# The second batch's gate products, moved from two blocks at the end of attention into slots of its last four steps

## The chip, the cores and the metric

The kernel runs on one core of one Trainium2 chip. The metric is the device time in microseconds of one execution. Before the change it is 691.11 us, the median of three runs (688.9 to 693.77).

## The reference, cut to what matters

Three layers follow one another: banded attention with four sink positions, a mixture of experts whose tokens are assigned greedily by gate logit, and a gated product.

```python
scores = scale * q @ k.T                       # B=2, H=8, S=768, D=64, window 128, 4 sinks
a = softmax(where(keep, scores, -1e9))
x = (a @ v)  -> (B*S, H*D) = (1536, 512)
logits = x @ w_gate                            # 512 x 8
# all (token, expert) pairs in order of falling logit; an expert takes 1536/8 = 192 tokens
out[mask_e] = relu(x[mask_e] @ w1[e]) @ w2[e]  # F = 1024
return ((y @ w_a) * (y @ w_b)) @ w_out         # d_ff = 1536
```

The logits need all 512 columns of a token's x, that is all four head pairs of its batch, and the assignment needs the logits of every token.

## The kernel before, in words

Attention is a loop over 48 steps, `t` from 0 to 47: 2 batches x 4 head pairs x 6 blocks of 128 queries. Head pair `g = t // 6` runs from 0 to 7; the last one, 7, is batch 1, pair 3, steps 42 to 47. Every engine has its own hand-ordered copy of this loop. On TensorE (`@block.tensor`) one turn `t` holds `transposes(t)` (the softmax rows of step t, L1222 and L1225), `scores(t + 2)` (L1209, absent in turns 46 and 47), `side_jobs(t, 0)`, `values(t - 1)` (eight records from L1244 and two from L1249: a 32-bit float product is two records of matmul and two of weight load), and `side_jobs(t, 1)`. A last turn 48 holds only `values(47)` and side jobs. VectorE finds the maxima of the scores (L761), copies half of the transposes (L791) and scales the values into `x_rows` (`keep_x`, L800). ScalarE takes the exponentials (L595), and copies the other half (L606, L610).

Side jobs are work for the next pair or for the gate. `side_list()` gives each a turn `t`, a place (0 ahead of `values`, 1 behind it), a kind and a half of the batch's 768 tokens. The kinds:

- `k`, `q`: turn the next pair's keys and queries (L1186).
- `rows`: turn three 128x128 tiles of `x_rows` with TensorE into bank 7 (L1276); ScalarE copies them to `xT` (L623).
- `gate`, `logits`: the first batch's product, `wg` (512x8) as the stationary operand and 384 columns of `xT` moving, then three small transposes back. They are not touched.
- `direct`: the second batch's product (L1258), `xT` tiles of 128x128 as the stationary operand and eight columns of `wg` moving. A half has three token tiles and four blocks of 128 input columns (one per head pair), 12 products in all; half 0 sums in bank 0, half 1 in bank 1. VectorE copies each half to `L` (L818).

The two semaphores `side_ready` (TensorE to the reader) and `side_done` (reader to TensorE) count the jobs in the order of the list; TensorE waits for `side_done` of every earlier job before it starts one, since they share bank 7. `SIDES` is their number.

At the end of attention before the change: `direct` half 0 stands in turn 47 behind `values(46)` with all 12 products, and right behind it TensorE issues the first three blocks of half 1, 9 products, without a wait. That is one run of 21 products ahead of `values(47)`. Turn 48: `values(47)`, `rows` of pair 7 half 1, then `direct` half 1 with the last block, three products.

Behind this the routing begins. VectorE waits for `side_done` = `SIDES`, sums `|L|` (L899), and runs a chain with small products on TensorE (L1324, L1332, L1336), which ends in the token order; GpSimd gathers the rows by it, and TensorE starts the experts (L1406, L1407). GpSimd's constants (L502 to L509) and two weight loads on SyncE (L400, expert 1, units 2 and 3) also wait for `SIDES`. SyncE stores `x_rows` of each pair (L394).

Of the kernel before, what the change touches and what calls it, by code (L numbers as in the profile page):

```python
# [5 lines left out]
def attention_moe_gated_product_kernel(  # L6
# [17 lines left out]
    ACT = mybir.ActivationFunctionType  # L24
    AX = mybir.AxisListType

    P = 128
# [3 lines left out]
    E = w_gate.shape[1]  # L31
# [5 lines left out]
    NBLK = S // P  # L37
    NPAIR = H // 2
    NCH = N // P
    KD = DM // P  # L40
# [31 lines left out]
    with ctx:  # L72
# [3 lines left out]
        def sem(name):  # L76
            return ctx.enter_context(nc.semaphore(name))
# [14 lines left out]
        L = sb("L", [P, NCH, E], stack=early)  # L92
# [25 lines left out]
        xT = sb("xT", [P, KD, S], stack=attn)  # L118
        wg = sb("wg", [P, KD, E], stack=attn)
# [65 lines left out]
        bank = [psum[:, i, :] for i in range(8)]  # L185
# [18 lines left out]
        side_done = sem("side_done")  # L204
# [8 lines left out]
        pts_done = sem("pts_done")  # L213
        o_ready = sem("o_ready")
        x_kept = sem("x_kept")

        dve_step = sem("dve_step")
        abs_ready = sem("abs_ready")
# [53 lines left out]
        HS = S // 2  # L272
# [6 lines left out]
        STEPS_A = B * NPB  # L279
        PAIRS = B * NPAIR  # L280

        def side_list():

            jobs = []
            for g in range(PAIRS):
                t = NBLK * g
                if g + 1 < PAIRS:
                    jobs += [(t + 1, 1, "k", g + 1, 0), (t + 2, 0, "k", g + 1, 1),
                             (t + 2, 1, "q", g + 1, 0), (t + 3, 0, "q", g + 1, 1)]
                jobs += [(t + 4, 0, "rows", g, 0)]  # L290
                if g + 1 < PAIRS:
                    jobs += [(t + 7, 0, "rows", g, 1)]
                    if g % NPAIR == NPAIR - 1:
                        jobs += [(t + 6, 0, "gate", g, 0), (t + 9, 1, "logits", g, 0),
                                 (t + 11, 0, "gate", g, 1), (t + 12, 0, "logits", g, 1)]
            last = PAIRS - 1
            return sorted(jobs) + [(STEPS_A - 1, 1, "direct", last, 0), (STEPS_A, 1, "rows", last, 1),
                                   (STEPS_A, 1, "direct", last, 1)]

        SIDES = len(side_list())  # L300

        def side_number(kind, g, half):
            return [job[2:] for job in side_list()].index((kind, g, half))
# [152 lines left out]
        def _(pool):  # L456
# [41 lines left out]
                nc.gpsimd.tensor_tensor(ring_lo[u][:, :], raw[u][:, :], ring[u][:, :].bitcast(f32),  # L498
                                        ALU.subtract).then_inc(w_lo[u], 1)

            pool.wait_ge(side_done, SIDES)
            nc.gpsimd.memset(thr[:, 0, :], -BIG)  # L502
            nc.gpsimd.memset(thr[:, 1, :], 0.0)
            nc.gpsimd.iota(tid[:], pattern=[[P, NCH], [0, E]], base=1, channel_multiplier=1,
# [62 lines left out]
        def _(act):  # L567
# [45 lines left out]
            def side_jobs(t, late):  # L613
                for no, (at_t, at_late, kind, g, half) in enumerate(side_list()):
                    if (at_t, at_late) != (t, late) or kind not in ("k", "q", "rows"):
                        continue
                    act.wait_ge(side_ready, no + 1)
                    if kind == "k":
                        round_k(bank[7], g, half).then_inc(rounded, 1)
                    elif kind == "q":  # L620
                        round_q(bank[7], g, half).then_inc(rounded, 1)
                    else:
                        nc.scalar.activation(xT[:, g % NPAIR, half * HS:(half + 1) * HS], bank[7][:, 0:HS],  # L623
                                             ACT.Copy).then_inc(side_done, 1)

            def round_ahead(t):

# [103 lines left out]
        def _(dve):  # L731
# [72 lines left out]
            def side_jobs(t, late):  # L804
                for no, (at_t, at_late, kind, g, half) in enumerate(side_list()):
                    if (at_t, at_late) != (t, late) or kind == "rows":
                        continue
                    dve.wait_ge(side_ready, no + 1)
                    c0 = g // NPAIR * NBLK + 3 * half
                    if kind == "k":  # L810
                        split_k(bank[7], g, half, rounds_before(kind, g, half)).then_inc(side_done, 1)
                    elif kind == "q":
                        split_q(bank[7], g, half, rounds_before(kind, g, half)).then_inc(side_done, 1)
                    elif kind == "gate":
                        nc.vector.tensor_copy(LT[:, half * HS:(half + 1) * HS], bank[7][0:E, 0:HS]).then_inc(side_done, 1)
                    else:
                        src = bank[half] if kind == "direct" else bank[7]
                        nc.vector.tensor_copy(L[:, c0:c0 + 3, :], src[:, 0:3 * E].rearrange("p (i e) -> p i e", e=E)  # L818
                                              ).then_inc(side_done, 1)

            nc.vector.memset(spin[:], 1.0).then_inc(spin_ready, 1)
# [72 lines left out]

            dve.wait_ge(rconsts, 1)

            dve.wait_ge(side_done, SIDES)
            at(dve_step, 0)
            nc.vector.tensor_reduce(out=absum[:], in_=L[:], axis=AX.XY, op=ALU.add,  # L899
                                    apply_absolute_value=True).then_inc(abs_ready, 1)  # L900
# [3 lines left out]
            for d in range(1, E):  # L904
                op = nc.vector.tensor_tensor(ties[:, :, o:o + E - d], L[:, :, d:E], L[:, :, 0:E - d], ALU.is_equal)
# [17 lines left out]
            with dve.Fori(0, STEPS) as st:  # L923
# [12 lines left out]
                for c in range(NCH):  # L936

                    op = nc.vector.tensor_scalar(above[:, c, :], bucket[:], um[:, c:c + 1], None, op0=ALU.is_le)  # L938
# [51 lines left out]
            with dve.If(even_v == 0):  # L990
# [20 lines left out]
                with dve.Fori(0, ROUNDS) as r:  # L1011
# [9 lines left out]
                    for c in range(NCH):  # L1021
                        gb = c % 4
                        if c >= 4:
# [3 lines left out]
                        op = nc.vector.scalar_tensor_tensor(out=G[:, gb, own], in0=mrow[:, own],  # L1027
                                                            scalar=m[:, c:c + 1], in1=tielt[:], op0=ALU.subtract,
                                                            op1=ALU.is_lt)
                        if c > 0:  # L1030

                            op = nc.vector.tensor_scalar(G[:, gb, 0:c * P], mrow[:, 0:c * P], m[:, c:c + 1], None,
                                                         op0=ALU.is_lt)
                        if c < NCH - 1:
                            op = nc.vector.tensor_scalar(G[:, gb, (c + 1) * P:N], mrow[:, (c + 1) * P:N],
                                                         m[:, c:c + 1], None, op0=ALU.is_le)
# [140 lines left out]
        def _(pe):  # L1177
# [72 lines left out]
                                            skip_group_check=True)  # L1250
                last.then_inc(o_ready, 1)

            def direct(half, blocks):

                for t in blocks:
                    for i in range(3):
                        at = (3 * half + i) * P
                        op = nc.tensor.matmul(bank[half][:, i * E:(i + 1) * E], xT[:, t, at:at + P], wg[:, t, :],  # L1258
                                              start=(t == 0 and i == 0), stop=(t == KD - 1), skip_group_check=True)
                return op  # L1260

            def side_jobs(t, late):
                for no, (at_t, at_late, kind, g, half) in enumerate(side_list()):
                    if (at_t, at_late) != (t, late):
                        continue

                    if no == 0:
                        pe.wait_ge(first_lo, 4)
                    pe.wait_ge(side_done, no)
                    b, pr = divmod(g, NPAIR)  # L1270
                    hs = slice(half * HS, (half + 1) * HS)
                    if kind == "rows":

                        pe.wait_ge(x_kept, NBLK * g + 3 * half + 3)
                        for i in range(3):
                            op = nc.tensor.transpose(bank[7][:, i * P:(i + 1) * P],  # L1276
                                                     x_rows[:, b * NBLK + 3 * half + i, pr * P:(pr + 1) * P], ident[:])
                    elif kind == "gate":
                        if b == 0 and half == 0:
                            pe.wait_ge(wg_in, 16)  # L1280
                        for blk in range(KD):
                            op = nc.tensor.matmul(bank[7][0:E, 0:HS], wg[:, blk, :], xT[:, blk, hs], start=(blk == 0),  # L1282
                                                  stop=(blk == KD - 1))
                    elif kind == "logits":
                        for i in range(3):
                            op = nc.tensor.transpose(bank[7][:, i * E:(i + 1) * E],
                                                     LT[:, half * HS + i * P:half * HS + (i + 1) * P], ident[0:E, 0:E])
                    elif kind == "direct":
                        op = direct(half, range(KD) if half == 0 else range(KD - 1, KD))
                    else:  # L1290
                        if half == 0:
                            pe.wait_ge((q_in, k_in)[kind == "k"][pr], 32 * (b + 1))
                        op = transposed(bank[7], (q_raw, k_raw)[kind == "k"], pr, half)
                    op.then_inc(side_ready, 1)
                    if kind == "direct" and half == 0:
                        direct(1, range(KD - 1))

            pe.wait_ge(spin_ready, 1)
            spinning(14, bank[0])
# [13 lines left out]
            for t in range(1, STEPS_A + 1):  # L1313
# [5 lines left out]
                values(t - 1)  # L1319
                side_jobs(t, 1)  # L1320


            pe.wait_ge(abs_ready, 1)
            nc.tensor.matmul(bank[0][:, 0:1], ones[:], absum[:], start=True, stop=True).then_inc(abs_summed, 1)  # L1324
# [205 lines left out]
```

## Time and profile before

| what | us |
|---|---|
| median of three runs | 691.11 |
| the profiled execution, its own time | 689.06 |
| its span, first to last instruction | 687.3 |
| outside the span | 1.76 |
| attention, to the end of the last `values` | about 168 |
| routing, to the first expert product | about 168 to 231 |
| experts and gated product | 231 to 687 |

The span is what the profile shows in detail; the 1.76 us around it is taken as it is. "Granted clock" is the share of TensorE's full clock that it ran at in a stretch; its two levels here are 1.00 (2.4 GHz) and 0.50 (1.2 GHz). PE is the matmul row of TensorE and PEld its weight-load row. The end of a matmul is modelled, so the distance from one start to the next says more than the duration of one record.

### The profile page before, as it was taken

To read this page: it belongs to the slowest core of one execution; us is meant where nothing else is said; L and a number is where in the kernel's file an instruction comes from. 1 tells how busy PE (TensorE), PEld (TensorE's weight loads), DVE (VectorE), ACT (ScalarE), POOL (GpSimd) and SP (SyncE) were. 2 spreads that over 40 slices of the span, in tenths; PEclk is the share of its full clock that TensorE was granted. 3 is DMA by queue.
4 is the path that set the end of the run, shared out by engine and by line. 5 is a ranking of instruction groups with operands and counts; after the bars stand their busy time and mean duration, and the time that the engine had idled before them with its cause. 6 is when DMAs were issued, how large, how long until landed. Compare 5 with 4: busy or idle time off the path is not lost.

```text
span 687.3 us, 10549 instructions
## 1 busy us (share of the span) xinstructions
PE 622.6 (91%) x3666; PEld 529.3 (77%) x3666; DVE 328.6 (48%) x979; ACT 301.5 (44%) x685; POOL 136.8 (20%) x74
## 2 busy tenths in 40 slices
PE   7999999999212699999999999999999999999995
PEld 4877776788111699999999888888888888888884
DVE  4677656761886187777777522212221213222221
ACT  3676665660000177777777433323342415141411
POOL 3000000000000602222222005050613223441402
PEclk8999999996555699999999999999999999999999
DMA  9954150220300636766676505050604131523001
GB/s 191 265 130 92 48 169 24 85 87 23 122 0 3 184 95 214 233 207 233 244 229 199 184 0 184 0 184 2 242 17 166 51 132 61 183 73 110 0 0 61
DMA packets 85812, 81.22 MB, mean 118 GB/s; under 512 B 39697, under 2 KB 62225, under 8 KB 85777
## 3 DMA queue, kind: packets, MB, share of 16 engines
q1 hardware_dynamic: 83856, 74.49, 36.2%
q0 software_dynamic: 1920, 6.29, 2.7%
q8 instruction: 19, 0.31, 0.2%
q14 instruction: 17, 0.13, 0.1%
HBM read 74.48 MB, written 6.29 MB: 118 GB/s over the span
## 4 chain that ended last, share of the span: by engine, by line
PE 85%; DVE 8%; issue 2%; ACT 2%; POOL 1%; DMA 1%; DVEq 0%; ACTq 0%; POOLq 0%
PE psum L1406 15%; PE psum L1399 15%; PE psum L1400 14%; PE psum L1401 14%; PE psum L1407 7%; PE psum L1244 5%; PE psum L1222 3%; PE psum L1209 3%; PE psum L1249 2%; DVE above L938 2%; PE psum L1186 2%; PE psum L1258 1%; PE psum L1276 1%; PE psum L1390 1%; PE psum L1282 1%
## 5 line engine op out<-in xcount | busy, mean ns | idle before, releaser
L498 POOL TENSOR_TENSOR w_lo<-w_raw,w_hi 128x2048 fp32r<-128x2048 f32 x23 | 106.5, 4646 | 298.3 <-ACT w_hi L575 298.3
L575 ACT ACTIVATE w_hi<-w_raw 128x1024 fp32r<-128x1024 f32 (+1 forms) x126 | 123.5, 999 | 18.7 <-PE psum L1401 18.7
L1150 DVE TENSOR_TENSOR g_sb<-psum,a_sb 128x512 f32<-128x512 f32 x36 | 24.9, 692 | 197.0 <-PE psum L1401 197.0
L1399 PE MATMUL psum<-y_hi,w_hi 128*128 x288 | 113.1, 393 | 0.0
L1401 PE MATMUL psum<-y_hi,w_lo 128*128 x288 | 112.2, 389 | 0.0
L1400 PE MATMUL psum<-y_lo,w_hi 128*128 x288 | 112.1, 389 | 0.0
L735 DVE TENSOR_TENSOR w_lo<-w_raw,w_hi 128x1024 fp32r<-128x1024 f32 x64 | 77.8, 1215 | 0.0
L1406 PE MATMUL psum<-x_hl,w_hi 128*128 (+1 forms) x256 | 75.2, 365 | 1.6 <-DVE x_hl L1100 1.6
L1406 PE MATMUL psum<-h_hl,w_hi 128*128 128x384 f32 x256 | 74.6, 361 | 0.0
L1407 PE MATMUL psum<-x_hl,w_lo 128*128 (+1 forms) x256 | 64.7, 253 | 0.0
L1399 PEld LDWEIGHTS psum<-y_hi,w_hi 128*128 128x128 f32 x288 | 54.0, 188 | 13.5 <-POOL w_lo L498 2.5
L1407 PE MATMUL psum<-h_hl,w_lo 128*128 128x192 f32 x256 | 64.1, 250 | 0.0
L1401 PEld LDWEIGHTS psum<-y_hi,w_lo 128*128 128x128 f32 x288 | 54.1, 188 | 11.4
L708 ACT ACTIVATE g_hi<-g_sb 128x512 fp32r<-128x512 f32 x36 | 22.8, 632 | 91.1 <-DVE g_sb L1150 91.1
L1400 PEld LDWEIGHTS psum<-y_lo,w_hi 128*128 128x128 f32 x288 | 54.1, 188 | 11.0
L702 ACT ACTIVATE a_sb<-psum 128x512 f32<-128x512 f32 x36 | 21.5, 598 | 88.2 <-PE psum L1401 88.2
L1399 PE MATMUL psum<-w_hi,g_hi 128*128 128x512 f32 x144 | 56.9, 395 | 0.0
L1400 PE MATMUL psum<-w_lo,g_hi 128*128 128x512 f32 x144 | 56.1, 390 | 0.0
L1401 PE MATMUL psum<-w_hi,g_lo 128*128 128x512 f32 x144 | 56.0, 389 | 0.0
L595 ACT ACTIVATE p_sb<-psum,nmax 128x264 f32<-128x264 f32 (+1 forms) x96 | 43.4, 459 | 21.3 <-DVE nmax L761 21.3
L1406 PEld LDWEIGHTS psum<-x_hl,w_hi 128*128 128x128 f32 x256 | 48.9, 191 | 2.0 <-issue 2.0
L1407 PEld LDWEIGHTS psum<-x_hl,w_lo 128*128 128x128 f32 x256 | 49.7, 194 | 0.0
(154 smaller groups left out, 998.3 us busy)
## 6 DMA issues: line engine op xcount, KB each, us to landing
w_raw<-in_moe_w_dram SPq DMA_DIRECT2D x32, 1024.0 KB, 5.1
w_raw<-in_moe_w_a_dram SPq DMA_DIRECT2D x9, 1024.0 KB, 5.2
w_raw<-in_moe_w_b_dram SPq DMA_DIRECT2D x9, 1024.0 KB, 5.1
w_raw<-in_moe_w_out_dram SPq DMA_DIRECT2D x9, 1024.0 KB, 5.5
k_raw<-in_k_dram SPq DMA_DIRECT2D x16, 192.0 KB, 3.8
q_raw<-in_q_dram SPq DMA_DIRECT2D x16, 192.0 KB, 4.0
v_sb<-in_v_dram SPq DMA_DIRECT2D x16, 192.0 KB, 4.2
xs_scratch<-x_rows SPq DMA_DIRECT2D x8, 384.0 KB, 3.6
```

The source lines that it names most:

```text
L498: nc.gpsimd.tensor_tensor(ring_lo[u][:, :], raw[u][:, :], ring[u][:, :].bitcast(f32), ALU.subtract).then_inc(w_lo[u], 1)
L575: op = nc.scalar.activation(ring[slot][:, ps], raw[r][:, ps], ACT.Copy)
L595: op = nc.scalar.activation(p_sb[:, t % 2, h * SW:(h + 1) * SW][:, span(t, h)], bank[2 * (t % 2) + h][:, span(t, h)], ACT.Exp, scale=-1.0, ...
L708: nc.scalar.activation(g_hi[:, j % 2, :], g_sb[:, j % 2, :], ACT.Copy).then_inc(g_hi_done, 1)
L735: op = nc.vector.tensor_tensor(ring_lo[slot][:, hs], raw[slot][:, hs], ring[slot][:, hs].bitcast(f32), ALU.subtract)
L1150: nc.vector.tensor_tensor(g_sb[:, j % 2, :], bank[2 + j % 2][:, :], a_sb[:, j % 2, :], ALU.mult).then_inc(g_prod, 1)
L1244: last = nc.tensor.matmul(o[:, h * D:(h + 1) * D], pT[:, t % 2, blk, h, :], v_sb[:, pr, i - 1 + blk, h, :], start=(h == 0 and blk == t0), ...
L1399: nc.tensor.matmul(o, lhs_hi, rhs_hi, start=first, stop=False)
L1400: nc.tensor.matmul(o, lhs_hi, rhs_lo, start=False, stop=False)
L1401: return nc.tensor.matmul(o, lhs_lo, rhs_hi, start=False, stop=final)
L1406: nc.tensor.matmul(bk[:, 0:2 * CAP], lhs_hi, rhs_both, start=first, stop=False)
L1407: return nc.tensor.matmul(bk[:, 0:CAP], lhs_lo, rhs_hi, start=False, stop=final)
```

## The change

The 24 products stay, with the same operands. What changes is where they stand and where they sum:

- All 24 sum in bank 7, columns 0 to 23 for half 0 and 24 to 47 for half 1 (`last_gate`).
- 21 of them go in seven groups of three into turns 44 to 47, by the table `LAST_GATE` (turn, place) -> (half, block): (44,0), (44,1), (45,0), (45,1), (46,1), (47,0), and (47,1), which holds half 0's last block. The last three stand behind the loop, as before.
- `rows` of pair 7 use banks 0 and 1, which the scores have left, since bank 7 holds the sums.
- The two `direct` jobs leave the side list, so `SIDES` is smaller by two and is reached when ScalarE has copied the last rows. VectorE and GpSimd wait for a new semaphore `gate_ready` instead, set by the last product; SyncE keeps its wait for `SIDES`.
- VectorE copies both halves of `L` at once (128x48) behind `gate_ready`, and waits for that copy by `logits_kept`.

```diff
             last = PAIRS - 1
-            return sorted(jobs) + [(STEPS_A - 1, 1, "direct", last, 0), (STEPS_A, 1, "rows", last, 1),
-                                   (STEPS_A, 1, "direct", last, 1)]
+            return sorted(jobs + [(STEPS_A, 1, "rows", last, 1)])
...
+        LAST_GATE = {(STEPS_A - 4, 0): (0, 0), (STEPS_A - 4, 1): (0, 1), (STEPS_A - 3, 0): (0, 2),
...
+        def rows_bank(g, half):
+            return half if g == PAIRS - 1 else 7
...
-            pool.wait_ge(side_done, SIDES)
+            pool.wait_ge(gate_ready, 1)
...
-            dve.wait_ge(side_done, SIDES)
+            dve.wait_ge(gate_ready, 1)
+            nc.vector.tensor_copy(L[:, NCH - NBLK:NCH, :], bank[7][:, 0:NBLK * E].rearrange("p (i e) -> p i e", e=E)
+                                  ).then_inc(logits_kept, 1)
+            dve.wait_ge(logits_kept, 1)
...
-            def direct(half, blocks):
-
-                for t in blocks:
-                    for i in range(3):
-                        at = (3 * half + i) * P
-                        op = nc.tensor.matmul(bank[half][:, i * E:(i + 1) * E], xT[:, t, at:at + P], wg[:, t, :],
-                                              start=(t == 0 and i == 0), stop=(t == KD - 1), skip_group_check=True)
+            def last_gate(half, blk):
+
+                for i in range(3):
+                    at = (3 * half + i) * P
+                    op = nc.tensor.matmul(bank[7][:, (3 * half + i) * E:(3 * half + i + 1) * E], xT[:, blk, at:at + P],
+                                          wg[:, blk, :], start=(half == 0 and blk == 0 and i == 0),
+                                          stop=(blk == KD - 1), skip_group_check=True)
                 return op
...
-                    if kind == "direct" and half == 0:
-                        direct(1, range(KD - 1))
+                if (t, late) in LAST_GATE:
+                    half, blk = LAST_GATE[t, late]
+                    pe.wait_ge(side_done, side_number("rows", PAIRS - 1 if blk == KD - 1 else PAIRS - 2,
+                                                      0 if blk == KD - 1 else 1) + 1)
+                    last_gate(half, blk)
...
+            pe.wait_ge(side_done, SIDES)
+            last_gate(1, KD - 1).then_inc(gate_ready, 1)
```

TensorE's rows of turn 44 before (softmax transposes, scores of step 46, values of step 43):

```order
L1222 MATMUL psum<-ident,p_sb 128x128 [waits pts_done,ptA_done,p_ready]
L1222 MATMUL psum<-ident,p_sb 128x128
L1225 MATMUL psum<-ident,p_sb 8x128
L1222 MATMUL psum<-ident,p_sb 128x128 [waits ptB_done]
L1222 MATMUL psum<-ident,p_sb 128x128
L1209 MATMUL psum<-k_hi,q_hi 128x264 [waits p_ready]
L1209 MATMUL psum<-k_hi,q_hi 128x264
L1209 MATMUL psum<-k_lo,q_hi 128x264 x2
L1209 MATMUL psum<-k_hi,q_lo 128x264 x2
L1244 MATMUL psum<-v_sb,pT 128x64 [waits x_kept,ptB_done,ptA_done]
L1244 MATMUL psum<-v_sb,pT 128x64 x3
L1249 MATMUL psum<-v_sink,pTs 128x128 [waits pts_done]
```

The same turn with the change, from its last scores on to the first transpose of turn 45 (L1219 are the scores, L1254 and L1259 the values, L1232 the transposes, ten lines further down than before):

```order
L1219 MATMUL psum<-k_lo,q_hi 128x264 x2
L1219 MATMUL psum<-k_hi,q_lo 128x264 x2
L1267 MATMUL psum<-wg,xT 128x8 [waits side_done]
L1267 MATMUL psum<-wg,xT 128x8 x2
L1254 MATMUL psum<-v_sb,pT 128x64 [waits x_kept,ptB_done,ptA_done]
L1254 MATMUL psum<-v_sb,pT 128x64 x3
L1259 MATMUL psum<-v_sink,pTs 128x128 [waits pts_done]
L1267 MATMUL psum<-wg,xT 128x8 [waits side_done]
L1267 MATMUL psum<-wg,xT 128x8 x2
L1232 MATMUL psum<-ident,p_sb 128x128 [waits pts_done,ptA_done,p_ready]
```

Two groups of three products have come into the turn, one on each side of the values. Turn 45 has two as well, turn 46 one, turn 47 two.

TensorE's rows at the end of attention before, from the end of `values(46)`:

```order
L1249 MATMUL psum<-v_sink,pTs 128x128 [waits pts_done]
L1258 MATMUL psum<-wg,xT 128x8 [waits side_done]
L1258 MATMUL psum<-wg,xT 128x8 x20
L1244 MATMUL psum<-v_sb,pT 128x64 [waits x_kept,ptB_done,ptA_done]
L1244 MATMUL psum<-v_sb,pT 128x64 x3
L1249 MATMUL psum<-v_sink,pTs 128x128 [waits pts_done]
L1276 MATMUL psum<-ident,x_rows 128x128 [waits x_kept,side_done]
L1276 MATMUL psum<-ident,x_rows 128x128 x2
L1258 MATMUL psum<-wg,xT 128x8 [waits side_done]
L1258 MATMUL psum<-wg,xT 128x8 x2
```

And with the change:

```order
L1259 MATMUL psum<-v_sink,pTs 128x128 [waits pts_done]
L1267 MATMUL psum<-wg,xT 128x8 [waits side_done]
L1267 MATMUL psum<-wg,xT 128x8 x2
L1254 MATMUL psum<-v_sb,pT 128x64 [waits x_kept,ptB_done,ptA_done]
L1254 MATMUL psum<-v_sb,pT 128x64 x3
L1259 MATMUL psum<-v_sink,pTs 128x128 [waits pts_done]
L1286 MATMUL psum<-ident,x_rows 128x128 [waits x_kept,side_done]
L1286 MATMUL psum<-ident,x_rows 128x128 x2
L1267 MATMUL psum<-wg,xT 128x8 [waits side_done]
L1267 MATMUL psum<-wg,xT 128x8 x2
```

The run of 21 products ahead of `values(47)` has become one of three; what stands behind it is in the same order as before.

## Rows read from the trace of the kernel before

**Rows 1.** The page's granted clock, in 40 slices of the span.

```profile
PEclk8999999996555699999999999999999999999999
```

**Rows 2.** The chain of work that ended last: start us, length us, what.

```profile
157.71 7.75 PE psum L1258 x42
...
168.09 0.30 DVE x_rows L800
...
169.43 0.50 ACT xT L623
...
171.75 0.25 DVE absum L899
```

**Rows 3.** The timeline, turns 43 to 47: start us, us, engine, line, what [idle before].

```profile
147.15 0.31 PEld L1276 LDWEIGHTS psum<-ident,x_rows 128*128 128x128 f32 x3
...
147.74 0.49 ACT L623 ACTIVATE xT<-psum 128x384 f32<-128x384 f32 x1 [0.73 <-PE psum L1276]
...
149.13 0.97 PEld L1244 LDWEIGHTS psum<-v_sb,pT 128*128 128x128 f32 x8
...
150.58 0.20 PEld L1222 LDWEIGHTS psum<-ident,p_sb 128*128 128x128 f32 x2
...
151.28 0.19 PEld L1209 LDWEIGHTS psum<-k_hi,q_hi 64*128 64x128 f32 x2 [0.17 <-issue]
...
151.84 0.97 PEld L1244 LDWEIGHTS psum<-v_sb,pT 128*128 128x128 f32 x8
...
153.29 0.20 PEld L1222 LDWEIGHTS psum<-ident,p_sb 128*128 128x128 f32 x2
...
156.19 0.97 PEld L1244 LDWEIGHTS psum<-v_sb,pT 128*128 128x128 f32 x8
...
157.23 0.29 PEld L1249 LDWEIGHTS psum<-v_sink,pTs 8*128 8x128 f32 x2
...
157.82 0.29 DVE L800 TENSOR_TENSOR x_rows<-psum,rden 128x128 f32<-128x128 f32 x1 [0.98 <-PE psum L1249]
```

**Rows 4.** The timeline behind the run of products.

```profile
165.24 1.83 PEld L1244 LDWEIGHTS psum<-v_sb,pT 128*128 128x128 f32 x8
...
167.19 0.50 PEld L1249 LDWEIGHTS psum<-v_sink,pTs 8*128 8x128 f32 x2
...
168.49 0.50 PEld L1276 LDWEIGHTS psum<-ident,x_rows 128*128 128x128 f32 x3 [0.81 <-issue]
...
169.97 1.35 PEld L1258 LDWEIGHTS psum<-wg,xT 128*128 128x128 f32 x6 [0.98 <-ACT xT L623]
...
171.46 0.18 DVE L818 COPY L<-psum 128x24 f32<-128x24 f32 x1 [3.08 <-PE psum L1258]
171.67 1.00 SPq L400 DMA_DIRECT2D w_raw<-in_moe_w_dram  x2
```

**Rows 5.** L1258 alone in two stretches: PE and PEld busy (records touched), granted clock, DMA.

```profile
157.64:159.12 1.48, 1.48 (x13) 1.48 (x14) 1.00 0.00 0
159.12:165.24 6.12, 6.12 (x31) 6.12 (x30) 0.50 0.00 0
```

**Rows 6.** TensorE in stretches: PE busy (records), granted clock, DMA share, GB/s.

```profile
131.80:135.20 3.40, 2.62 (x20) 1.00 0.63 230
...
155.70:159.10 3.40, 3.40 (x28) 1.00 0.00 0
...
234.00:235.00 1.00, 1.00 (x8) 0.90 0.76 201
12.00:13.00 1.00, 0.03 (x2) 0.67 1.35 224
19.00:20.00 1.00, 1.00 (x11) 0.92 1.35 220
```

**Rows 7.** The timeline near the program's start.

```profile
18.29 0.28 PEld L1209 LDWEIGHTS psum<-k_hi,q_hi 64*128 64x128 f32 x2 [0.33 <-issue]
...
19.23 0.31 PEld L1186 LDWEIGHTS psum<-ident,k_raw 128*128 128x128 f32 x3 [0.23 <-issue]
```

More of the change, by code:

```diff
@@ L215, in attention_moe_gated_product_kernel @@
         x_kept = sem("x_kept")
+        gate_ready = sem("gate_ready")
+        logits_kept = sem("logits_kept")
         dve_step = sem("dve_step")
@@ L296, in side_list @@
             last = PAIRS - 1
-            return sorted(jobs) + [(STEPS_A - 1, 1, "direct", last, 0), (STEPS_A, 1, "rows", last, 1),
-                                   (STEPS_A, 1, "direct", last, 1)]
+            return sorted(jobs + [(STEPS_A, 1, "rows", last, 1)])
         SIDES = len(side_list())
+        LAST_GATE = {(STEPS_A - 4, 0): (0, 0), (STEPS_A - 4, 1): (0, 1), (STEPS_A - 3, 0): (0, 2),
+                     (STEPS_A - 3, 1): (1, 0), (STEPS_A - 2, 1): (1, 1), (STEPS_A - 1, 0): (1, 2),
+                     (STEPS_A - 1, 1): (0, KD - 1)}
+        def rows_bank(g, half):
+            return half if g == PAIRS - 1 else 7
         def side_number(kind, g, half):
@@ L622, in side_jobs @@
                     else:
-                        nc.scalar.activation(xT[:, g % NPAIR, half * HS:(half + 1) * HS], bank[7][:, 0:HS],
-                                             ACT.Copy).then_inc(side_done, 1)
+                        nc.scalar.activation(xT[:, g % NPAIR, half * HS:(half + 1) * HS],
+                                             bank[rows_bank(g, half)][:, 0:HS], ACT.Copy).then_inc(side_done, 1)
             def round_ahead(t):
@@ L816, in side_jobs @@
                     else:
-                        src = bank[half] if kind == "direct" else bank[7]
-                        nc.vector.tensor_copy(L[:, c0:c0 + 3, :], src[:, 0:3 * E].rearrange("p (i e) -> p i e", e=E)
+                        nc.vector.tensor_copy(L[:, c0:c0 + 3, :], bank[7][:, 0:3 * E].rearrange("p (i e) -> p i e", e=E)
                                               ).then_inc(side_done, 1)
@@ L1275, in side_jobs @@
                         for i in range(3):
-                            op = nc.tensor.transpose(bank[7][:, i * P:(i + 1) * P],
+                            op = nc.tensor.transpose(bank[rows_bank(g, half)][:, i * P:(i + 1) * P],
                                                      x_rows[:, b * NBLK + 3 * half + i, pr * P:(pr + 1) * P], ident[:])
@@ L1287, in side_jobs @@
                                                      LT[:, half * HS + i * P:half * HS + (i + 1) * P], ident[0:E, 0:E])
-                    elif kind == "direct":
-                        op = direct(half, range(KD) if half == 0 else range(KD - 1, KD))
                     else:
```

## The prediction

> **What bounds the kernel now.** I read the granted clock of the whole span first, then the chain of waits, the timeline of the end of attention, and last the stretches with their clock. The clock row [rows 1] shows TensorE near full clock in attention, low in the slices of the routing, and full again to the end. The chain [rows 2] shows what the change touches: 7.75 us of L1258 in 42 records, which is the run of 21 products, then `values(47)`, the scaling at 168.09, the last rows on ScalarE at 169.43, and the first sum of the routing at 171.75. Everything behind it is one dependent sequence (VectorE's routing, the gather, the experts), so what is gained or lost up to 171.75 goes to the end of the span.
>
> Turns 44 to 47 are bounded by TensorE itself [rows 3]: turn 45 begins at 150.58, its scores at 151.28, its values at 151.84, turn 46 at 153.29, and the reader is to see that the only gap printed is 0.17 us of issue, not a wait for another engine. So a product put into these turns finds no room; it pushes what follows it.
>
> The second thing to see is the clock. The run starts at 157.64 at full clock and loses it at 159.12 [rows 5]. TensorE was busy for all of 155.70 to 159.10 and the clock still fell, while in 131.80 to 135.20 it was busy for 2.62 of 3.40 us and the clock held [rows 6]. So here an unbroken busy row did not protect the clock. What the engine did before it fell was turns 46 and 47, which have no scores, and then 1.48 us of products that move eight columns each behind a full weight load.
>
> **The change part by part.** Durations come from the profiled execution, 689.06 us with a span of 687.3; the sum is made against it. The median of the runs shown is 2.05 us above it.
>
> *The price of a group.* In the first stretch of the run, 1.48 us hold 12 to 13 records: 0.118 us each, 0.71 a group of three products (six records). In the second, 6.12 us hold 29 to 30: 0.207 each, 1.24 a group [rows 5].
>
> *The run goes.* It takes 157.64 to 165.24, 7.60 us. Seven groups at full clock cost 7 x 0.71 = 4.97, and all of it stays on the path: six groups push the values and transposes behind them, the seventh stands ahead of `values(47)`. Gain 2.63.
>
> *The tail, if the clock holds.* From the first weight load of the values to the scaling is 1.63 at full clock (156.19 to 157.82) [rows 3] and 2.85 in the low one (165.24 to 168.09) [rows 2, 4]: 1.22. From the first rows transpose to ScalarE's copy, 0.59 (147.15 to 147.74) against 0.94 (168.49 to 169.43): 0.35 [rows 2 to 4]. The last group, 1.24 against 0.71: 0.53. Together 2.10. With the clock held to the end the change would give 2.63 + 2.10 = 4.73.
>
> *The clock, if it falls early.* The ratio of low to full is 1.75 for these products [rows 5], 1.88 for the values (165.24 to 167.19 against 156.19 to 157.23) [rows 3, 4] and 1.68 for the scores (18.29 to 19.23 against 151.28 to 151.84) [rows 3, 7]. I take 1.77, near the middle: each microsecond of the held-clock schedule that is run low costs 0.77 more. In that schedule the first group starts at 149.13, where the values of turn 44 start now [rows 3]; the others end at 152.0, 154.0, 156.1, 159.2, 160.5 and 162.6 (the old starts plus 0.71 for each earlier group). A fall at F costs 0.77 x (162.6 - F) plus the 2.10 of the tail that is then not saved. It balances at 162.6 - 2.63/0.77 = 159.2.
>
> When does it fall? Turns 44 and 45 took 2.7 us (150.58 to 153.29) and now hold 1.42 us more of the same thin products, a third of their time; turn 46 and 47 lose density from the missing scores as before and get three groups on top. The only fall that the trace has under a busy TensorE came 1.48 us into such products. The bounds for F are therefore 150.6 (as long behind the first group's start) and never. I take 154.0, behind the third group, since the first 1.48 us of thin work are then interleaved with scores, which the case of rows 5 did not have, and three groups (2.1 us) have passed. That costs 0.77 x 8.6 = 6.6 in the turns, and the tail's 2.10 are not saved; against the 4.73 it leaves +4.0.
>
> The Trainium skill, "TensorE: Matmul & The Clock Gate", section "Why this matters for your kernels", asks to avoid throughput drops by leaving no idle gaps between bursts of matmuls. By that rule nothing here loses the clock, for the moved groups leave no gap, and the sum would be -4.7; the trace does not agree, since the clock fell at 159.12 with the row 3.40 of 3.40 us busy [rows 6].
>
> *The copy.* One copy of 128x48 stands in place of 128x24 at 0.18 us [rows 4], behind the same semaphore step. Its bounds: nothing, and 0.11, the difference to the 128x128 read of a bank at 0.29 [rows 3]. I take 0.05.
>
> *Moved at no cost.* The waits for `side_done` in the groups: ScalarE's copy for block 2 starts at 147.74 and takes 0.49 [rows 3], over before 149.13, where the first group stands; block 3's rows are copied in turn 46, some 5 us ahead of the group in turn 47. Behind these waits stand the values; were ScalarE late, they would be late by as much. Banks 0 and 1 are free of scores from turn 46 on. SyncE's two loads now wait for ScalarE's rows copy instead of VectorE's: about 1.7 us ahead of 171.67, relative to the path [rows 4]; they feed the experts some 60 us later, so it neither gains nor costs. GpSimd's constants wait for the same moment as before, and are not on the path.
>
> Sum: -2.63 (the run) - 2.10 (the tail) + 2.10 (tail not saved) + 6.6 (low clock in turns 45 to 47) + 0.05 = +4.0, so 689.06 + 4.0 = 693.1 us, 0.6% slower: less than the 1% or so that a measurement of this kernel can tell from no change.
>
> One unknown comes with any shift: the low stretch in which the experts begin, 231 to 234.2 [rows 6]. Nothing or the length of the first low stretch (12.3 to 19.2, 6.9 us) are its bounds; half of it is lost time, so -1.5 to +1.9.
>
> **The rivals.**
>
> *The clock falls as late as before*, in the last group (161.9). For it: the scores, denser work, still stand between the groups in turns 44 and 45. Against: two groups in each of these turns, and no scores in turns 46 and 47. 0.77 x 0.7 = 0.5, so 0.5 + 2.10 - 4.73 = -2.1: 687.0.
>
> *It never falls before the routing*: -4.7, 684.3. For it, the stretch at 131.80, which kept the clock with a gap. Against it, `values(47)` is followed by waits for VectorE and ScalarE at the same thin load.
>
> *It falls at once and everything is priced at the highest ratio*, slower by over 1%. Place: 150.6, in turn 44; price 0.88 x 12.0 = 10.6; 10.6 + 2.10 - 4.73 = +8.0: 697.1. It decides from a fall before about 151.8 at this ratio. For it: 1.48 us sufficed at 157.64. Against: a turn with scores had just passed.
>
> *The change moves work but not the end*, within 1 us of 689.1: a fall near 159.2, where loss and gain balance.
>
> **How the numbers follow.** Clock lost in turns 44 to 46 (F from 151 to 158, +0.9 to +6.3): 0.56. As late as before: 0.20. Balanced: 0.10. Never: 0.05. At once, highest ratio: 0.09. The predicted time is the first case's 693.1. The range takes in the late fall, 687.0 less 0.5, and on the other side 697.1, with 1 us for the 2.05 by which the median lies above the profiled execution: 686.5 to 698. Only the dearest case, or a lower one that meets a long low stretch at the experts, is slower by over 1% (6.9 us): 0.09. Faster by over 1% needs the never case and 1.5 us at the experts with luck besides: 0.02. Within 1%: 0.89.
>
> **What would show it.** In the profile after: the granted clock is 0.50 from some point between 151 and 158 on, and turns behind it take 1.7 to 1.9 times as long; `values(47)` starts behind a group of six records; the first sum of the routing starts near 175.8 instead of 171.75. Wrong: a clock of 1.00 up to 160 and beyond, with the first sum at 167 to 170; or an idle time printed ahead of the groups or the values, which would mean a wait that I priced at nothing.

## The result, and the profile after

| | kernel before | changed kernel |
|---|---|---|
| median, 20 runs each | 690.93 us | 695.96 us |
| lowest and highest | 688.6 to 695.42 | 689.97 to 708.2 |
| the profiled execution | 689.06 | 695.96 |
| its span | 687.3 | 694.2 |

The ratio is 1.0059, 95% interval 1.0033 to 1.0085: slower by 0.6%, as forecast (4.0 us, 0.6%), and inside the 1% to which the forecast gave a chance of 0.89. Two executions of the changed kernel ran in a slower state (708 us), and the ratio leaves them out. The medians differ by somewhat more than the ratio says, 5.0 us.

The chain of waits of the changed kernel, over the end of attention (start us, length us, what), answers to [rows 2]:

```profile
151.00 0.77 PE psum L1267 x6
...
153.12 0.77 PE psum L1267 x6
...
155.04 0.77 PE psum L1267 x6
...
157.71 1.38 PE psum L1267 x6
...
163.21 1.38 PE psum L1267 x6
...
165.75 1.08 PE psum L1267 x6
...
169.35 1.38 PE psum L1267 x6
170.73 1.80 PE psum L1254 x8
...
173.36 0.30 DVE x_rows L808
...
175.25 1.46 PE psum L1267 x6
...
177.04 0.25 DVE absum L909
```

The run of 42 records at 7.75 us has become seven pieces of six, and no other engine stands between them. The first three take 0.77 us, the later ones up to 1.38. The reason is in the stretches of the same profile (PE busy, granted clock, DMA share, GB/s), which answer to [rows 6]:

```profile
155.00:156.00 1.00, 1.00 (x11) 1.00 0.00 0
156.00:157.00 1.00, 1.00 (x8) 0.68 0.00 0
157.00:158.00 1.00, 1.00 (x4) 0.50 0.00 0
...
241.00:242.00 1.00, 1.00 (x7) 0.65 0.86 242
```

With TensorE busy throughout, the clock fell at 156.36 (0.68 in that microsecond is 0.36 of it at 1.00 and the rest at 0.50), behind the third group, and stayed at 1.2 GHz until 241.7 (0.65 is 0.7 of that microsecond at 0.50).

A mark is needed that all kernels share. I use the one weight load of eight columns that each turn from the second block of a pair on has (L1225 before, L1235 after). In the kernel before, turns 44 to 47:

```profile
148.05 0.09 PEld L1225 LDWEIGHTS psum<-ident,p_sb 128*8 128x8 f32 x1
...
150.75 0.09 PEld L1225 LDWEIGHTS psum<-ident,p_sb 128*8 128x8 f32 x1
...
153.46 0.09 PEld L1225 LDWEIGHTS psum<-ident,p_sb 128*8 128x8 f32 x1
...
155.78 0.09 PEld L1225 LDWEIGHTS psum<-ident,p_sb 128*8 128x8 f32 x1
```

In the changed kernel:

```profile
149.84 0.09 PEld L1235 LDWEIGHTS psum<-ident,p_sb 128*8 128x8 f32 x1
...
153.88 0.09 PEld L1235 LDWEIGHTS psum<-ident,p_sb 128*8 128x8 f32 x1
...
159.19 0.13 PEld L1235 LDWEIGHTS psum<-ident,p_sb 128*8 128x8 f32 x1
...
164.69 0.13 PEld L1235 LDWEIGHTS psum<-ident,p_sb 128*8 128x8 f32 x1
```

Turn 44, all at full clock, grew from 2.70 to 4.04 us, 1.34 for two groups. Turn 45 grew to 5.31 and turn 46, all at the low clock and with one group, from 2.32 to 5.50.

The 6.9 us between the two spans divide so. Ahead of the mark, 1.79 (149.84 against 148.05): this execution had a low stretch of 3.4 us from 57.4 on, in code that the change does not touch, and later kernels have such a stretch or not irrespective of their end of attention. From the mark to the first routing sum, 27.20 against 23.70: +3.50, the change. From that sum to the first expert product, 59.55 against 59.37: +0.18. From there to the end, 457.6 against 456.2: +1.4, of which about 1.0 is that the experts began with 5.1 us at the low clock instead of 3.1 (half of 2.0). So one profile alone would have charged the change with twice its price; the stretch from the mark to the first sum is what the experiments are read by.

### The profile page after: what moved, and what is told of

The parts are those of the page before. It is cut to its first block, busy times and chain, and to the rows that moved or that the text cites. A ratio compares the mean times of both kernels' runs of the same rounds, so it can differ in the third digit from the quotient of the medians.

```text
span 694.2 us, 10548 instructions
## 1 busy us (share of the span) xinstructions
PE 629.1 (91%) x3666; PEld 534.7 (77%) x3666; DVE 328.8 (47%) x978; ACT 301.6 (43%) x685; POOL 136.7 (20%) x74
## 4 chain that ended last, share of the span: by engine, by line
PE 85%; DVE 8%; issue 2%; ACT 2%; POOL 1%; DMA 1%; DVEq 0%; ACTq 0%; POOLq 0%
PE psum L1420 15%; PE psum L1413 14%; PE psum L1415 14%; PE psum L1414 14%; PE psum L1421 7%; PE psum L1254 6%; PE psum L1232 3%; PE psum L1219 3%; PE psum L1259 2%; PE psum L1196 2%; DVE above L948 2%; PE psum L1267 1%; PE psum L1286 1%; PE psum L1404 1%; PE psum L1191 1%
## 5 line engine op out<-in xcount | busy, mean ns | idle before, releaser
L1414 PEld LDWEIGHTS psum<-y_lo,w_hi 128*128 128x128 f32 x288 | 54.1, 188 | 11.1
```

The source lines that it names most:

```text
L1414: nc.tensor.matmul(o, lhs_hi, rhs_lo, start=False, stop=False)
```

## The experiments

My theory was that the thin products (128x8 behind a full 128x128 weight load), spread among the last turns, take the clock early, and that this is the whole loss. The rivals: the bank, the wider copy or the new waits cost it; or a product put into these turns costs by its place. This table has every profile of the study; "fall" is the granted clock's fall counted from turn 44's mark, "stretch" is mark to first routing sum, "ratio" is to the kernel before in the same comparison. Each comparison has its own runs of the kernel before, which is why its median is 690.93 in one and 693.97, 693.77 or 693.2 in the others.

| kernel | fall, us | stretch, us | ratio (95% interval) |
|---|---|---|---|
| before | 11.1 | 23.70 | 1 |
| changed | 6.5 | 27.20 | 1.0059 (1.0033 to 1.0085) |
| changed, again | 4.2 | 29.18 | 1.0041 (1.0006 to 1.0076) |
| e1, one run, bank 7 | 11.0 | 23.77 | 1.0000 (0.9970 to 1.0030) |
| e3, turns 46 and 47 only | 10.2 | 24.25 | 1.0016 (0.9989 to 1.0043) |
| e2, one wide matmul per group | 16.8 | 20.34 | 0.9996 (0.9964 to 1.0028) |
| e2, two per group | 20.2 | 20.69 | 1.0003 (0.9970 to 1.0036) |
| e4, wide form | 16.9 | 20.91 | 0.9959 (0.9923 to 0.9994) |
| e10, wide form again | 16.9 | 20.96 | 0.9950 (0.9925 to 0.9975) |
| e5, wide form, tail filled | 17.9 | 21.33 | 0.9981 (0.9943 to 1.0018) |
| e6, e5 and gather filled | 16.7 | 22.33 | 0.9929 (0.9894 to 0.9964) |
| e11, e6 again | 17.9 | 21.29 | 0.9907 (0.9873 to 0.9941) |
| e7, before, gather filled | 10.0 | 24.71 | 0.9953 (0.9920 to 0.9986) |
| e8, before, wide matmuls in the run | 13.3 | 22.99 | 1.0000 (0.9971 to 1.0029) |

How far one profile can be trusted shows where the work up to the first routing sum is the same. The kernel before and e7 gave 23.70 and 24.71; e5, e6 and e11 gave 21.33, 22.33 and 21.29; e4 and e10 gave 20.91 and 20.96; the changed kernel gave 27.20 and 29.18. So a difference of up to 1 us between two single profiles is no difference of the kernels by itself, unless the clock fell at the same place in both. In e7 the end of attention is that of the kernel before, and yet the clock fell about 1 us earlier:

```profile
159.54 8.71 PEld L1258 LDWEIGHTS psum<-wg,xT 128*128 128x128 f32 x42
```

```profile
159.00:160.00 1.00, 1.00 (x8) 0.96 0.00 0
```

The run of thin products begins at 159.54 and the clock falls at 159.9, 0.4 us into it, where it had been 1.5 us.

**All groups back in one run (e1).** Only the table and its use differ from the changed kernel.

```diff
-        LAST_GATE = {(STEPS_A - 4, 0): (0, 0), (STEPS_A - 4, 1): (0, 1), (STEPS_A - 3, 0): (0, 2),
...
+        LAST_GATE = {(STEPS_A - 1, 1): ((0, 0), (0, 1), (0, 2), (0, 3), (1, 0), (1, 1), (1, 2))}
...
+                for half, blk in LAST_GATE.get((t, late), ()):
```

> The changed kernel with all seven groups (21 products) back in turn 47 behind values(46), but still summing in bank 7, with rows of pair 7 in banks 0 and 1, one copy of L and the new semaphores. Theory (the low clock in turns 44 to 47 is the whole loss): the clock falls about 1.5 us into the run as in the kernel before, the first sum of the routing stands within 0.5 us of that kernel's place counted from turn 44, and the time is that of before, 690 to 692, ratio 0.998 to 1.002. Rival (the bank, the wider copy or the waits cost the time): it stays near the changed kernel, 694 to 697, ratio 1.004 to 1.008.

Measured: 693.95 us against 693.97 for before, ratio 1.0000. Its chain of waits:

```profile
157.64 7.78 PE psum L1265 x42
...
168.06 0.30 DVE x_rows L806
...
169.95 1.46 PE psum L1265 x6
...
171.74 0.25 DVE absum L907
```

These are the times of [rows 2] to within 0.07 us, and here the clock fell at the same place as well (11.0 against 11.1 us behind the mark), so the two profiles can be compared directly. The bank, the copy of 128x48, `gate_ready` and the banks of the last rows cost at most 0.1 us; that rival falls. What is left of the change is where the seven groups stand.

**Groups in turns 46 and 47 only (e3).** One behind the values of turn 46, one ahead of those of turn 47, five behind them.

```diff
+        LAST_GATE = {(STEPS_A - 2, 1): ((0, 0),),
+                     (STEPS_A - 1, 0): ((0, 1),),
+                     (STEPS_A - 1, 1): ((0, 2), (0, 3), (1, 0), (1, 1), (1, 2))}
```

> The groups leave turns 44 and 45: one in turn 46 (behind the values), one in turn 47 ahead of the values, five in turn 47 behind them. Theory (what counts is how early thin products stand among the turns with scores): the clock falls only around the run in turn 47, as before, and the time is that of before within 1.5 us, ratio 0.997 to 1.002. Rival (any spreading costs by itself, by a stall that each group brings): a third to a half of the loss of 5 us stays, 692.5 to 694.

Measured: ratio 1.0016, stretch 24.25, fall at 10.2. The stretch is 0.55 above the kernel before and 2.95 below the changed one. The ratio lies in the range that the theory expected, but its interval does not exclude the rival's 1.7 to 2.5 us. The stretch is no longer than that of e7 (24.71), and the fall, 0.9 us earlier than in the kernel before, is no earlier than there. So no loss from these groups is seen, and the stretch speaks for the theory.

**One wide matmul behind each group (e2).** The groups stay exactly where the change has them.

```diff
                     last_gate(half, blk)
+                    for no in range(1):
+                        nc.tensor.matmul(bank[7][:, 64:512], spin[:, 0:P], spin[:, 0:448], start=False, stop=False,
+                                         skip_group_check=True)
```

> The changed kernel with one extra matmul of 448 bf16 columns of ones behind each of the seven groups, into unused columns of bank 7; nothing reads them. Each is 0.19 us at full clock by its columns, 1.3 in all. Theory (thin groups take the clock): one may not be enough; where it holds until the last group, 690.9 - 4.7 + 1.3 = 687.5 at best; if it falls only in turn 47, 689 to 691. Rival (the moved groups cost by their place, not by the clock): the changed kernel's 695.9 and 1.3 more, 697.

The chain of waits of that kernel, and its clock:

```profile
153.34 0.77 PE psum L1267 x6
...
157.65 0.77 PE psum L1267 x6
...
160.74 0.77 PE psum L1267 x6
...
170.30 0.25 DVE absum L909
```

```profile
160.00:161.00 1.00, 1.00 (x8) 1.00 0.00 0
...
165.00:166.00 1.00, 1.00 (x10) 1.00 0.00 0
166.00:167.00 1.00, 0.51 (x3) 0.90 0.00 0
```

The groups keep their 0.77 us to the end and the clock falls at 166.8, behind `values(47)`. The stretch is 20.34: 6.9 us shorter than the changed kernel, with seven more matmuls in it. This shows the mechanism: in the same places the same products cost 6.9 us less when the clock holds. The forecast of -4.7 + 1.3 = -3.4 against the kernel before is met in the stretch (20.34 - 23.70 = -3.36), but partly by balance: turn 44 took 4.30 us against 4.04, so a wide matmul added 0.13 us and not 0.19, while the last rows and the last group ran at the low clock. The whole time missed the forecast: 691.77 is above the 691 expected, and the ratio of 0.9996 has an interval that does not reach the 0.995 expected at best. Where the 3 us of the stretch went in the whole time is not known.

**Two wide matmuls per group (e2).** The loop above with `range(2)`.

> As the run with one extra matmul per group, but two, 2.6 us of extra work at full clock. Theory: the granted clock is 1.00 through turns 44 to 47, the first sum of the routing comes 22.6 - 4.7 + 2.6 = 20.5 us behind the place of the first group (2.1 more if the clock falls ahead of values(47)), and the time is 688.8 to 691, that is 5 to 7 us below the changed kernel though it does more work. Rival (not the clock): 695.9 + 2.6 = 698.5.

Measured: 693.73, ratio 1.0003, above the 691 expected and below the rival's 698.5. The clock held through all of the stretch. From the first group, at 163.00, to the first routing sum, at 182.60, it is 19.6 us, 0.9 less than the 20.5 expected; the stretch from the mark is 20.69. Against the one wide matmul per group the second bought nothing. The profiled execution (701.89) had 34 us at the low clock in the first turns and two more low stretches ahead of its turn 44, so I read only its stretch behind the mark.

**The same work in a wide form (e4, e10).** No idle filler; three of four blocks change the operand that moves, and six small products are added that bring the sums back. The places change a little too: one wide product in each of (44,0), (44,1), (45,0) and (46,1), none in (45,1), and two in (47,0).

```diff
+            def wide_gate(half, blk):
+                bk = bank[1 if half else 7]
+                op = nc.tensor.matmul(bk[0:E, 0:HS], wg[:, blk, :], xT[:, blk, half * HS:(half + 1) * HS],
+                                      start=(blk == 0), stop=(blk == KD - 2))
...
+            def back(half):
+                pe.wait_ge(wide_kept, half + 1)
+                for i in range(3):
+                    at = (3 * half + i) * P
+                    nc.tensor.matmul(bank[7][:, (3 * half + i) * E:(3 * half + i + 1) * E], LT[:, at:at + P],
+                                     ident[0:E, 0:E], start=(half == 0 and i == 0), stop=False, skip_group_check=True)
```

> The changed kernel, but the first three blocks of each half in the form that the first batch has: 8 columns of wg stationary and 384 columns of xT moving, two records of 0.32 us each by their columns. Half 0 in turns 44 and 45 (bank 7), half 1 in turns 46 and 47 (bank 1); VectorE copies each to LT, and three small products bring it back to bank 7, where the last block is added as before. The result is the same sum. Six wide products at 0.64 are 3.8 us, six small ones 0.7, one group 0.7: 5.3 against the 5.0 of seven thin groups. Theory (thin products take the clock, not the place): the clock holds to turn 47 or beyond, first group to first routing sum 19 to 20.5 us against 26.1 in the changed kernel, time 2 to 4 us below the kernel before. Rival (any product put among these turns costs its stalls, whatever its form): no better than the changed kernel, 26 us and 5 us above before.

Measured: 690.26 against 693.77, ratio 0.9959 (0.9923 to 0.9994). The timeline of its weight loads in turns 44 and 45:

```profile
150.15 0.09 PEld L1242 LDWEIGHTS psum<-ident,p_sb 128*8 128x8 f32 x1
...
151.25 0.10 PEld L1281 LDWEIGHTS psum<-xT,wg 128*8 128x8 f32 x2
151.99 0.97 PEld L1261 LDWEIGHTS psum<-v_sb,pT 128*128 128x128 f32 x8 [0.65 <-ACT pT L616]
...
153.44 0.10 PEld L1281 LDWEIGHTS psum<-xT,wg 128*8 128x8 f32 x2
154.18 0.20 PEld L1239 LDWEIGHTS psum<-ident,p_sb 128*128 128x128 f32 x2 [0.65 <-issue]
154.35 0.09 PEld L1242 LDWEIGHTS psum<-ident,p_sb 128*8 128x8 f32 x1
```

A wide product takes 0.74 us (151.25 to 151.99), no less than the thin group's 0.66 to 0.77, and turn 44 is 4.20 us long, longer than the 4.04 of the changed kernel. It is not cheaper in its place; yet the stretch is 20.91 against 27.20, since the clock fell only at 167.1. From the first wide product to the first routing sum it is 19.8 us (151.25 to 171.06), inside the 19 to 20.5 expected. That rules out the rival that any product among these turns costs by its place.

> The wide form a second time, to tell its gain from the spread of the runs. Theory: the stretch is 20 to 21.5 us again and the ratio to before 0.993 to 0.998. Rival: the first result was luck in other stages, ratio 0.998 to 1.002.

Measured: 689.12 against 693.2, ratio 0.9950 (0.9925 to 0.9975), stretch 20.96. The gain holds. In all five profiles of this form (e4, e10, e5, e6, e11) the clock outlasted the last turns and fell within 1.3 us of the first of the three small products that follow `values(47)`.

**The waits of the tail filled (e5).** Two extra matmuls of 448 columns behind `values(47)` and its three small products, four behind the last rows.

```diff
                     back(1)
+                    filled(2, bank[3], 448)
...
+            filled(4, bank[3], 448)
             pe.wait_ge(side_done, SIDES)
```

> As the wide form, with two extra matmuls of 448 columns of ones (bank 3, read by nobody) behind values(47) and four behind the last rows transposes, where TensorE waits for VectorE and ScalarE. Theory: if the clock would fall in these last 5 us, up to 2.1 us are saved, on average half of it; nothing is lost, since the waits there are 0.5 to 1 us each. Rival: the extra work stands in the way, and the end comes 0.3 to 1 us later than in the wide form.

Measured: 0.9981, stretch 21.33, 0.4 longer than the wide form. Its TensorE timeline in the tail:

```profile
165.33 0.55 PE L1297 MATMUL psum<-spin 128*128 128x448 bf16 x2
165.72 0.70 PE L1313 MATMUL psum<-ident,x_rows 128*128 128x128 f32 x3
166.21 1.70 PE L1297 MATMUL psum<-spin 128*128 128x448 bf16 x4
167.71 1.29 PE L1274 MATMUL psum<-wg,xT 128*128 128x8 f32 x6
```

The clock fell at 165.9 all the same, behind the first two; the four that follow then took 1.5 us at the low clock, and the last group had to wait for them: it began at 167.7, 0.75 us after the copy of the last rows had ended (166.46 + 0.49). 0.4 us alone would be inside the spread of equal profiles, but this delay can be read directly, and the stretches of the same tail in e6 and e11, 22.33 and 21.29, also lie above the wide form's 20.9. So the rival was right for these six matmuls. They came late, though: here four of the six began after the fall, and in e6, where the clock fell at 166.3, all six did (from 167.4 on). Whether filler that starts earlier would hold it was not tested.

**The wait for the gather filled (e6, e11, e7).**

```diff
+            gather_fill(14)
             for s in range(2):
                 turn_x(s, 4 + s)
+            gather_fill(4)
```

> As the run before it, with 14 extra matmuls of 512 bf16 columns of ones while TensorE waits for the gathered rows, and 4 behind the first two tiles' transposes. Theory: the experts begin at full clock instead of 3.1 us (kernel before) or 4.8 us (changed kernel) at the low one, which saves half of that, 1.5 to 2.4 us more. Rival: the clock falls again in the short wait behind the transposes, or the extra work delays them: no gain, or up to 0.5 us lost.

> The wide form with both waits filled, a second time. Theory: ratio to before 0.990 to 0.996 again, the lowest of all. Rival: no lower than the wide form alone.

Measured: 687.58 against 693.77, ratio 0.9929 (0.9894 to 0.9964), and again 687.38 against 693.2, ratio 0.9907 (0.9873 to 0.9941), the lowest of all. It beats the kernel before and the changed one. The intervals overlap with those of the wide form alone; what speaks for a further gain is that both medians lie lower, by 2.7 and 1.7 us. (The changed kernel's low stretch at the experts' start was 5.1 us, not the 4.8 of the expectation.) The same in the kernel before alone:

> The kernel before the change, with only the same extra matmuls in the wait for the gather. Theory: 1.5 to 2 us faster than before, ratio 0.997 to 0.998, by the low stretch of 3.1 us that goes at the experts' start; the end of attention stays as it is. Rival: same as before.

Measured: 689.86 against 693.77, ratio 0.9953 (0.9920 to 0.9986), that is 3.3 us, with an interval of 1 to 5.5 us that takes in the 1.5 to 2 expected. The clock was at full rate when the experts began, as the stretches of that kernel show (the wait and the first expert products):

```profile
228.00:229.00 1.00, 1.00 (x6) 0.90 0.85 229
...
234.00:235.00 1.00, 1.00 (x10) 1.00 0.75 205
```

But this one profile does not show where the gain lies. From first expert product to the end it took 456.7 us, against 456.2 in the kernel before, where 1.5 should have gone; e6 took 455.1 there. Profiles of kernels that are equal from the gather on differ there by 3 us and more (456.2 before, 460.3 in e1, which began the experts with 6.4 us at the low clock). That part of the spread is not explained.

**The kernel before, with wide matmuls in its run (e8).**

```diff
                                               start=(t == 0 and i == 0), stop=(t == KD - 1), skip_group_check=True)
+                    if half == 0 or t < KD - 1:
+                        nc.tensor.matmul(bank[7][:, 64:512], spin[:, 0:P], spin[:, 0:448], start=True, stop=True)
```

> The kernel before, its one run of 21 products in its old place, with one extra matmul of 448 columns of ones behind each three of them (into bank 7, read by nobody): 1.3 us more work at full clock. Theory (the clock is the price, the place is not): the clock outlasts the run, which takes 7 x (0.71 + 0.19) = 6.3 us instead of 7.6, and from turn 44's eight-column transpose to the first routing sum 22.4 us or less (20.4 if the tail is spared too) against 23.7; time 1.3 to 3 us below before. Rival (the run is bound by its own issue, or the clock falls all the same): 1.3 us or more above before, 25 us or more in that stretch.

Measured: ratio 1.0000, stretch 22.99. The chain of waits in the run:

```profile
159.50 0.77 PE psum L1258 x6
...
162.01 0.57 PE psum L1258 x6
...
163.79 1.08 PE psum L1258 x6
```

The clock fell at 163.2, 3.8 us into the run, where it had been 1.5 (before), 1.4 (e1) and 0.4 (e7). The 0.7 us by which the stretch is shorter than that of the kernel before lie inside the spread, and the ratio shows no gain. The expected hold to the end of the run did not come: one wide matmul for three thin products was enough among scores and values (e2) and not enough in a run without them. So the place seems to matter after all, by what stands around the thin products; this rests on one profile of each.

**The changed kernel once more (e9).**

> The changed kernel a second time, unaltered, for a second fall of the clock. Theory: the clock falls within turns 44 to 46, though not at the same instruction as in the first profile; the stretch from turn 44's eight-column transpose to the first routing sum is 25 to 29.5 us, longer by 0.77 us for each us that the fall is earlier; ratio to before 1.003 to 1.009. Rival (the first profile was a chance fall): the clock holds to turn 47 and the stretch is below 23.7.

Measured: 696.02 against 693.2, ratio 1.0041. The timeline of its weight loads, and its clock:

```profile
147.93 0.09 PEld L1235 LDWEIGHTS psum<-ident,p_sb 128*8 128x8 f32 x1
...
149.02 0.74 PEld L1267 LDWEIGHTS psum<-wg,xT 128*128 128x128 f32 x6
...
151.14 0.74 PEld L1267 LDWEIGHTS psum<-wg,xT 128*128 128x128 f32 x6
...
151.98 0.09 PEld L1235 LDWEIGHTS psum<-ident,p_sb 128*8 128x8 f32 x1
...
153.81 1.35 PEld L1267 LDWEIGHTS psum<-wg,xT 128*128 128x128 f32 x6 [0.24 <-issue]
```

```profile
151.00:152.00 1.00, 1.00 (x10) 1.00 0.00 0
152.00:153.00 1.00, 1.00 (x7) 0.54 0.00 0
```

The fall is at 152.1, behind the second group already, and the stretch is 29.18: 2.4 us earlier behind the mark (4.2 against 6.5) and 1.98 longer than in the first profile, about 0.84 for each microsecond. Both falls lie in turn 45, one at its start and one in its values. Two executions are all that was profiled: how often the clock falls so early, in runs that spread from 689.87 to 709.76 us, is not shown.

## Why the prediction was right

Point by point, by its own steps.

*TensorE bounds turns 44 to 47.* Right. In the chain of the changed kernel nothing but TensorE stands from 151.0 to 173.

*A group costs 0.71 us at full clock and 1.24 at the low one.* 0.67 (1.34 for two in turn 44), and at the low clock 1.23 to 1.28 from the group's first weight load to the values' (169.28 to 170.51, 165.33 to 166.61); the chain's 0.77 and 1.38 take in the modelled end. Turn 46 at the low clock was priced 2.32 x 1.77 + 1.24 = 5.35 and took 5.50.

*The clock falls in turns 44 to 46.* Right in both profiles. The step chose 154.0, which is 4.9 us behind the first group's start; measured 5.4 (150.93 to 156.36) and 3.1 (149.02 to 152.1).

*The sum.* From the first group's place to the first routing sum the kernel before takes 22.62 us (149.13 to 171.75). With the measured falls the prediction's formula gives 0.77 x 8.0 + 2.10 - 4.73 = +3.6 and 0.77 x 10.4 + 2.10 - 4.73 = +5.4; measured 26.11 and 28.09, that is +3.5 and +5.5. So the terms together were sized rightly, with the point of the fall as the only one that had to be chosen.

*Luck.* The 154.0 was a choice between 150.6 and never, and no row fixed it. On the same scale the falls came at 154.6 and 152.2, which is 1.8 us of time, and the 1.48 us of [rows 5] from which the lower bound was taken was 0.4 us in e7. That the early fall came was reasoned; that the sum met the ratio to 0.1 us is luck.

*The clock held would give 4.73.* Not seen for the changed kernel, but tested: held until the tail with seven extra matmuls, -3.36, and held throughout with fourteen, -3.01 (e2). The rival that rested on the rule of idle gaps (the Trainium skill, "TensorE: Matmul & The Clock Gate", "Why this matters for your kernels") does not describe this case: the clock fell at 156.36 and 152.1 with 1.00 of each microsecond busy. Busy is what the profile models, from a record's start to its modelled end; whether TensorE idles inside a thin product, and whether that is what takes the clock, no run here shows.

*The copy, 0.05.* From its start to the sum behind it, 0.24 us in the changed kernel (176.80 to 177.04) against 0.29 [rows 2, 4]. Nothing, by e1 too.

*Moved at no cost.* Right: no idle time ahead of the groups but 0.22 to 0.24 of issue at the low clock.

*The absolute time.* Forecast 693.1 from the profiled execution of 689.06; the median came at 695.96. The ratio agrees (0.58% forecast, 0.59% measured). Of the 2.9 us of difference 1.9 are the base, since the median of before lies that much above the execution that the sum was made against. The prediction said so of the three runs, and yet took the lower one. The other 1.0 is that the medians differ by 5.0 where 4.0 was forecast.

## What to carry to other kernels

Small products moved into the turns of the engine that bounds them are not free, and their length is the lesser part of the price: ask at which clock all that follows will run. Before thin matmuls are spread, see which turns the clock survives now and how near they are to losing it, and if the same sum can be had with the many columns moving and the few stationary, try that form even if it is no shorter in its place. To price such a change, take the distance between two marks around it in several profiles; the whole span mixes in low stretches that have nothing to do with it.

## What the runs showed of the hardware that I had not expected

The changed kernel lost its clock at two places 2.4 us apart, 6.5 and 4.2 us behind the same mark, and its first routing sum came 2.0 us later for it. The end of attention of the kernel before did the same on a smaller scale: 11.1 and 10.0 us, 23.70 and 24.71 (before, e7). A fully busy row kept or lost the clock by what it was busy with: thin products in a run lost it after 0.4 to 1.5 us (before, e1, e7), the same run with a wide matmul for every three after 3.8 (e8), and the same groups with wide matmuls among scores and values not before the tail (e2, 16.8 us). In the tail the clock fell before most of the wide filler ran (e5, e6), so what it could hold is open as well. Which property of the thin products takes the clock is open.
